# One-hot operations in step 0, both halves of the cluster dots in step 5, inverse sums once per head

## The reference

```python
q_assign = np.argmax(np.einsum('bhsd,hcd->bhsc', q_n, c_n), axis=-1)
k_assign = np.argmax(np.einsum('bhsd,hcd->bhsc', k_n, c_n), axis=-1)
mask = q_assign[:, :, :, None] == k_assign[:, :, None, :]
scores = scale * np.matmul(q, k.transpose(0, 1, 3, 2))
scores = np.where(mask, scores, -1000000000.0)
scores = scores - np.max(scores, axis=-1, keepdims=True)
attn = np.exp(scores)
attn = attn / (np.sum(attn, axis=-1, keepdims=True) + 1e-09)
return np.matmul(attn, v)
```

## Time and profile before

| | us |
|---|---|
| median of 3 runs | 837.04 (836.58 to 841.04) |
| the profiled execution | 836.16 |
| its span | 834.3 |
| TensorE busy in the span | 763.8 (92%) |
| VectorE busy | 611.2 (73%) |
| ScalarE busy | 458.1 (55%) |
| GpSimd busy | 357.4 (43%) |

### The profile page before, as it was taken

How to read it: one execution, slowest core, us unless ns; L and a number is a source line. 1 busy time by engine, 2 the same in 40 slices (tenths; PEclk the granted TensorE clock), 3 DMA queues, 4 the chain that set the end, 5 groups by cost and what they waited for, 6 DMA issues and landing times.

```text
span 834.3 us, 15672 instructions
## 1 busy us (share of the span) xinstructions
PE 763.8 (92%) x5407; PEld 715.3 (86%) x5408; DVE 611.2 (73%) x984; ACT 458.1 (55%) x865; POOL 357.4 (43%) x337
## 2 busy tenths in 40 slices
PE   3999999999999892299999999988999999999996
PEld 2899899989998882299999999987999999999995
DVE  2688888888888847156666667679987777778773
ACT  3677777777777752011111111137786776766762
POOL 5566757765665003604333355543232232313232
PEclk9999999999999996599999999999999999999999
DMA  8321111111200016416655456650000000000000
GB/s 243 81 49 29 39 28 47 28 38 28 48 35 1 0 50 220 136 27 227 210 191 169 160 179 223 201 202 1 1 13 14 1 26 1 26 0 25 0 26 25
DMA packets 67907, 63.59 MB, mean 76 GB/s; under 512 B 30872, under 2 KB 53528, under 8 KB 67872
## 3 DMA queue, kind: packets, MB, share of 16 engines
q1 hardware_dynamic: 65952, 56.85, 21.7%
q0 software_dynamic: 1920, 6.30, 2.0%
HBM read 56.32 MB, written 6.82 MB: 76 GB/s over the span
## 4 chain that ended last, share of the span: by engine, by line
PE 50%; issue 24%; DVE 13%; POOL 8%; ACT 3%; DMA 1%; POOLq 0%; DVEq 0%; SPq 0%; ACTq 0%
PE PS L502 8%; PE PS L503 8%; PE PS L504 8%; PE PS L381 7%; POOL HL L872 5%; PE PS L356 3%; PE PS L357 3%; PE PS L341 3%; PE PS L342 3%; PE PS L323 3%; DVE NM L924 2%; DVE PTL L985 1%; DVE w_low L969 1%; POOL out L881 1%; PE PS L365 1%
## 5 line engine op out<-in xcount | busy, mean ns | idle before, releaser
L502 PE MATMUL PS<-XH,w_high 128*128 128x256 f32 x640 | 183.2, 286 | 7.7 <-DVE XL L1149 3.6
L503 PE MATMUL PS<-XL,w_high 128*128 128x256 f32 x640 | 182.8, 286 | 0.0
L504 PE MATMUL PS<-XH,w_low 128*128 128x256 f32 x640 | 182.6, 285 | 0.0
L801 POOL TENSOR_SCALAR w_high<-w_raw 128x1024 fp32r<-128x1024 f32 x80 | 101.4, 1287 | 131.6 <-DMA w_raw<-in_moe_w 107.4
L872 POOL TENSOR_TENSOR HL<-U,HH 128x512 fp32r<-128x512 f32 x48 | 62.6, 1303 | 184.5 <-ACT HH L741 184.5
L502 PEld LDWEIGHTS PS<-XH,w_high 128*128 128x128 f32 x640 | 124.5, 195 | 10.6 <-issue 8.8
L985 DVE TENSOR_TENSOR PTL<-PS,PTH 128x384 fp32r<-128x384 f32 x192 | 98.5, 552 | 40.7 <-ACT PTH L650 40.7
L503 PEld LDWEIGHTS PS<-XL,w_high 128*128 128x128 f32 x640 | 124.5, 194 | 1.8
L504 PEld LDWEIGHTS PS<-XH,w_low 128*128 128x128 f32 x640 | 124.4, 194 | 0.0
L969 DVE TENSOR_TENSOR w_low<-w_raw,w_high 128x1024 fp32r<-128x1024 f32 x80 | 114.6, 1459 | 9.2 <-issue 9.2
L650 ACT ACTIVATE PTH<-PS 128x384 fp32r<-128x384 f32 x192 | 84.8, 489 | 47.0 <-PE PS L381 46.0
(11 more groups left out here) (171 smaller groups left out, 1726.6 us busy)
## 6 DMA issues: line engine op xcount, KB each, us to landing
w_raw<-in_moe_w SPq DMA_DIRECT2D x64, 512.0 KB, 7.9
xs<-xs_dram SPq DMA_DIRECT2D x9, 513.0 KB, 3.8
w_raw<-in_moe_w_in SPq DMA_DIRECT2D x8, 512.0 KB, 8.3
w_raw<-in_moe_w_out SPq DMA_DIRECT2D x8, 512.0 KB, 7.9
QK<-in_q SPq DMA_DIRECT2D x16, 192.0 KB, 3.1
QK<-in_k SPq DMA_DIRECT2D x16, 192.0 KB, 3.3
V<-in_v SPq DMA_DIRECT2D x16, 192.0 KB, 2.4
xs_dram<-zeros SPq DMA_DIRECT2D x1, 513.0 KB, 3.9
```

The lines of the kernel that those rows point to most:

```text
L502: nc.tensor.matmul(o, wh, xh, start=first, stop=False)
L503: nc.tensor.matmul(o, wh, xl, start=False, stop=False)
L504: return nc.tensor.matmul(o, wl, xh, start=False, stop=last)
L801: return nc.gpsimd.tensor_scalar(HIGH[par][:, p, :], RAW[par][:, p, :], 1.0, 0.0, ALU.mult, ALU.add)
```

## The change

VectorE does all five one-hot operations in step 0: two ahead of the normalisation and the low parts, three behind the maximum. The second half of the dots goes from step 0 to step 5 of the head before, behind the first half, and both ahead of `back`. The inverse sums of all six tiles are made together in step 5, in a buffer that has a half for each of two heads.

```diff
-        RS = esb("RS", [P, GT])
+        RS = esb("RS", [P, 2, JT])
...
@@ TensorE, steps
-                        if i == 0:
-                            if not far:
-                                prep_part(h + 1, 1 - par, 3)
+                        if i < 2:
                             if before:
-                                values(h - 1, 1 - par, 1, 0)
-                        elif i == 1:
-                            if before:
-                                values(h - 1, 1 - par, 1, 1)
+                                values(h - 1, 1 - par, 1, i)
...
                         else:
-                            back(h, 0)
                             if not end:
                                 prep_part(h + 2, par, 2)
+                                prep_part(h + 2, par, 3)
+                            back(h, 0)
...
             prep_part(1, 1, 2)
+            prep_part(1, 1, 3)
             steps(0, start=True)
...
@@ VectorE
+            def inverse_sums(g, par):
+
+                dve.wait_ge(exp_done, JT * (g + 1))
+                nc.vector.tensor_scalar(RS[:, par, :], SM[:, par, :], 1e-9, None, ALU.add).then_inc(rs_done, 1)
+                dve.wait_ge(rs_done, 2 * g + 1)
+                nc.vector.reciprocal(RS[:, par, :], RS[:, par, :]).then_inc(rs_done, 1)
+
+            def normalise(g, par, grp):
+                dve.wait_ge(rs_done, 2 * g + 2)
+                dve.wait_ge(back_done, HG * g + grp + 1)
...
                         if i == 0:
+                            if not far:
+                                one_hots(h + 1, 0)
+                                one_hots(h + 1, 1)
                             if before:
-                                normalise(h - 1, 0)
+                                normalise(h - 1, 1 - par, 0)
...
-                        if i < 2 and not far:
-                            for m in ((0, 1), (2, 3, 4))[i]:
-                                one_hots(h + 1, m)
                         if i < 4:
                             rowmax(h, par, i + 2)
                         elif not far:
                             rowmax(h + 1, 1 - par, i - 4)
-                        if before and i == 1:
-                            inverse_sums(h - 1, 1 - par, 1)
+                        if i == 0 and not far:
+                            for m in (2, 3, 4):
+                                one_hots(h + 1, m)
                         if before and i == 2:
-                            normalise(h - 1, 1)
-                        if i == 4:
-                            inverse_sums(h, par, 0)
+                            normalise(h - 1, 1 - par, 1)
+                        if i == 5:
+                            inverse_sums(h, par)
...
             steps(HEADS - 2, end=True)
-            normalise(HEADS - 1, 0)
+            normalise(HEADS - 1, 1, 0)
             early_logits(JT - 1)
-            inverse_sums(HEADS - 1, 1, 1)
-            normalise(HEADS - 1, 1)
+            normalise(HEADS - 1, 1, 1)
```

More of the change, by code:

```diff
@@ L945, in one_hots @@
                                             ALU.is_equal).then_inc(onehot_done, 1)
[L947 to L958, removed]
+            def inverse_sums(g, par):
[6 more added lines that the diff above has]
+                dve.wait_ge(back_done, HG * g + grp + 1)
                 nc.vector.tensor_tensor(XO[:, bass.ds(JT * (g // H) + GT * grp, GT), bass.ds(D * (g % H), D)],
                                         obank[:, 0:GT * D].rearrange("p (j d) -> p j d", d=D),
-                                        RS[:, :].unsqueeze(2).to_broadcast([P, GT, D]), ALU.mult).then_inc(xo_done, 1)
+                                        RS[:, par, GT * grp:GT * (grp + 1)].unsqueeze(2).to_broadcast([P, GT, D]), ALU.mult).then_inc(xo_done, 1)
             def early_logits(t):
```

## The result

| | before | after |
|---|---|---|
| median of 22 runs each, us | 838.40 | 841.69 (839.51 to 847.29) |
| ratio after to before | | 1.0045, 95% interval 1.0031 to 1.0059 |
| profiled execution, us | 836.16 | 839.86 |
| its span, us | 834.3 | 838.0 |
| one head, mean of twelve, us | 16.83 | 17.19 |

The change makes the kernel slower by 0.45%: 840.9 was forecast from 837.04, which is 1.0046. In the profile after, the lines of TensorE's steps keep their numbers and the others are lower. On VectorE, L921 is the maximum (L924 before), L931 and L933 the first two one-hot operations, L935, L937 and L939 the third to fifth, L947 and L949 the addition and the reciprocal of the inverse sums, L954 the normalisation, L983 the low parts. On GpSimd, L810 are the copies, L813 and L815 the low parts of the operands (L816 and L818 before), L825 the first part of the cut of the values (L828 before).

What follows compares the result with a forecast made beforehand. TensorE's order, 98% busy, was taken to set the pace. Thirteen heads +3.6, head 0 +1.0, head 14 -0.8, head 15 0: total +3.8 on the median 837.04 gave 840.9 us; range 829 to 847, likeliest case 838 to 843.5.

Steps and rivals of the forecast that it cites:

- The main step: VectorE, step 0: third one-hot operation, held by GpSimd's L818, ends 7.72 us after step 5's transposes start, instead of 6.95.
- the next T5: Start of the next head's step 5 transposes, forecast 17.10 us after this head's; before it was 16.82, 0.28 less.
- The page's rule: By the skill page, the held third one-hot operation would begin only at GpSimd's end: 0.15 more, 2 us above the forecast.
- The addition: Step 5, VectorE: the inverse sums' addition, held by GpSimd's fourth copy, takes 0.8 us instead of 0.16; TensorE doesn't feel it.
- The step that failed: Step 5: the way back stands 0.60 later, but its reader, the normalisation, comes at about +4.5 anyway, so it costs nothing.
- T1 stays at +5.75: TensorE's step 1 still starts 5.75 us after the start of step 5's transposes, as before the change.
- The head without any stall: A head without TensorE's 0.76 us wait at step 3 was put at 16.06 us instead of 16.82.
- B: Rival: the one-hot operations don't meet GpSimd; 0.50 us a head less, 829.5 us in all; chance 0.17.
- C: Rival: the fifth one-hot operation also meets GpSimd's L828; 0.7 us a head more, 850 us in all; chance 0.10.
- D: Rival: the stall at step 2 is as long as step 3's was, 0.76 us; 837.2 us in all; chance 0.10.
- E: Rival: the new 0.9 us wait in each head lowers TensorE's clock, some 1.5 us a head; 860 us; chance 0.03.
- L938 has a median of 1.1: Sign in the profile after: the third one-hot operation, in step 0, takes 1.1 us, ending 0.2 behind GpSimd's L818.

Runs made afterwards that it cites:

- f1: Kernel after, with the single pair of inverse sums moved from the end of step 5 to its start: 17.15 us a head, ratio to before 1.0026.
- f3: Kernel after, with inverse sums at the start of step 5 and AEQ in PSUM: 16.22 us a head, ratio to before 0.9869.
- e1: Kernel after, with AEQ in PSUM instead of SBUF: 17.09 us a head, ratio to before 1.0024.
- e5: Kernel before, with inverse sums made once a head, at the end of step 5: 17.30 us a head, ratio to before 1.0063.
- e2: Kernel after, with the normalisation of step 0 ahead of the first two one-hot operations: 17.18 us a head, ratio to before 1.0036.
- f2: Kernel after, with inverse sums at the start of step 5 and the normalisation first in step 0: 17.14 us a head, ratio to before 1.0047.

## Why the prediction was right, and where not

**The main step held in odd heads.** "Moved to step 0, the third operation ends at +7.72": measured +7.73. Its followers came at the forecast +8.15 and +8.43, step 2 at +9.04, the next T5 at +17.13 (forecast 17.10). In even heads the same +7.72 (169.59 - 161.87) is luck: the operation came so late by itself that from head 6 on it was held for 0.03 only, and without GpSimd it would have ended at about +7.69 (in head 2 it took 0.60, in head 4 it was not held). f1 against f3 shows that the meeting with L815 costs 0.93 a head where nothing else is late. In the kernel after, where other delays lie beside it, e1 shows that taking it away gives back 0.10.

**The page's rule.** By the Trainium skill, "SBUF — State Buffer", section Who interferes with whom, the loser of the shared ports blocks fully, and a VectorE instruction with at most one SBUF input does not contend outside the two-port modes; the place of AEQ in PSUM, which leaves one SBUF input, took the meeting away in every head of f3, and this trace agrees with the rule. The 0.35 that I read from it behind GpSimd's end did not come: the held operation ended 0.22 behind, and the rows' 0.20 was the better number.

**The addition** was held 0.8, as taken. That TensorE would not feel it was wrong.

**The step that failed** is the sentence on the way back and the normalisation: it "comes at about +4.5 anyway: nothing". I took the normalisation for a last reader. But the values of the next group write the same bank, and TensorE waits for it (`xo_done` in `values`) at T5 + 4.7. It also came later than I had it (about +4.5): it began at +4.85 and, in even heads, +5.27. VectorE stood idle for 0.20 to 0.24 ahead of it, and for 0.33 at the loop's turn, without waiting for anything that the profile shows; what filled this time no run shows. So "T1 stays at +5.75" became +6.47 and +6.84. The longer of two limits counts, so odd heads paid nothing for this and even ones some 0.14.

**The sum, term by term.** From the profiles, before to after: to the fifth step of head 0 +0.59 (forecast +1.0); the thirteen heads behind it 223.44 against 218.71, +4.7 (forecast +3.6; of the 1.1 that it missed, some 0.7 is the values' wait in the even heads, the rest that odd heads took 17.13 and not 17.10); head 14 -1.16 (forecast -0.8); head 15 -0.25 (0); the rest -0.2 (0). Together +3.7, forecast +3.8: the total owes its closeness partly to luck, to terms that cancel. The head without any stall was put at 16.06; f3, in which TensorE never stands in these heads, takes 16.22, so the stall of the kernel before was worth some 0.6 a head and not 0.76.

**Rivals.** B (829.5) was argued from no meeting; L935 met L815 in all heads, but paid for it mainly in the odd ones (0.82 against 0.38), and in head 4, starting 0.11 before L815's end, it took its own 0.35. f3 is roughly that world, at 16.22 a head (B had 16.32). C did not occur, L939 stayed at 0.36, but e5 shows the collision it named. D and E did not occur; the granted clock of the twelve heads stayed at 1.00.

**A number that was wrong** in the prediction, "L938 has a median of 1.1": it was 0.82 and 0.38 by turns, since it began later (at +6.91 and +7.34, not +6.6), with the same end.

## What to carry to other kernels

Before an operation is moved, look at what GpSimd does at its new place: an end set by the other engine doesn't move however early the operation is issued, and two places 3 us apart differed by 0.74 us in each head. List every reader and every next writer of a buffer whose release moves, and not only the one that the profile shows waiting today; it shows no wait that has slack. When delays lie side by side, taking away one shows almost nothing (0.10 in e1, 0.02 in e2 and 0.04 in f1, of 0.36 here), and only runs with the others out of the way give a price: 0.93 for the same edit as in e1. An end time that comes out as forecast does not show the mechanism; look whether the instruction is longer than it is alone.

## What the runs showed of the hardware

- A VectorE operation can lengthen a later one by way of GpSimd: AEQ in PSUM in the kernel before saved 0.22 us at an addition it doesn't touch (0.48 against 0.70), with 0.23 us less in GpSimd's L828.
- A two-input VectorE operation (L935) that GpSimd's low parts held ended 0.21 to 0.23 behind their end, however long it took in all (0.38 to 1.58 us in the kernel after, f1 and f2); the additions held in step 5 ended 0.02 to 0.04 behind GpSimd's copy.
- PSUM in place of SBUF cost the operations next to nothing: L935 356 ns on average, in SBUF 0.35 unheld.
- Not every VectorE operation meets GpSimd: beside L813, which ran from 148.52 on, the reciprocal L949 took 0.19 from 148.50 and left L813 at its usual 1.83, and the reduction L931 its 0.36 from 148.64.
- VectorE can stand idle behind short instructions (0.36) with nothing to wait for that the profile shows: 0.20 to 0.33 ahead of the normalisation, 0.33 to 0.38 at the loop's turn. In the kernel before, the normalisation stood behind a maximum of 0.95 and showed no idle time. Whether work of its own queue fills that time, no run shows.
